# Step 0 of a fused attention and two-layer kernel: order of weight loads, weight splitting, gram evictions and the second half's solve

## The reference, cut to what matters

```python
k_n = k / (norm(k) + 1e-6)                       # batch 4, heads 8, 768 tokens, head size 48
for t in range(768):
    y[t] = q[t] @ state
    state += beta[t] * outer(k_n[t], v[t] - k_n[t] @ state)
x = y as (3072 tokens, 384)
h = x @ w_in                                     # 384 -> 2048
g = where(h >= 1, h, where(h <= -1, 0, (h + 1)**2 / 4))
x = g @ w_out                                    # 2048 -> 384
xn = x / rms(x) * rms_g                          # second network: 384 -> 1536 -> 384, silu gate
out = (silu(xn @ w_gate) * (xn @ w_val)) @ w_out2
```

## Time and profile before

| what | value |
|---|---|
| median of 3 runs | 1063.65 us (1062.71 to 1069.65) |
| the profiled execution's own time | 1068.47 us |
| its span from first to last instruction | 1066.6 us |
| mean granted TensorE clock | 0.99 |
| TensorE busy | 1039.2 us, 97% |

### The profile page before, as it was taken

How to read it: one execution, slowest core, us unless ns; L and a number is a source line. 1 busy time by engine, 2 the same in 40 slices (tenths; PEclk the granted TensorE clock), 3 DMA queues, 4 the chain that set the end, 5 groups by cost and what they waited for, 6 DMA issues and landing times.

```text
span 1066.6 us, 25024 instructions
## 1 busy us (share of the span) xinstructions
PE 1039.2 (97%) x11132; PEld 856.3 (80%) x11132; DVE 535.0 (50%) x1001; ACT 468.8 (44%) x843; POOL 9.6 (1%) x20
## 2 busy tenths in 40 slices
PE   8889899999999999999999999999999999999996
PEld 4469888777777877777778888888888888888885
DVE  6648667747846837753356444324333333333322
ACT  5744654574473474464466542232232232232211
POOL 1000000000000000000000000000000000000000
PEclk9889999999999999999999999999999999999999
DMA  9405102301500410030021230200200100100101
GB/s 258 133 2 130 22 3 62 89 3 37 115 2 3 120 31 3 32 119 3 28 93 49 70 119 1 60 1 1 60 1 13 48 1 1 30 1 1 30 1 30
DMA packets 19034, 48.09 MB, mean 45 GB/s; under 512 B 2448, under 2 KB 9232, under 8 KB 17872
## 3 DMA queue, kind: packets, MB, share of 16 engines
q1 hardware_dynamic: 18800, 46.11, 16.0%
q10 hardware_dynamic: 128, 0.39, 0.1%
HBM read 37.06 MB, written 9.44 MB: 44 GB/s over the span
## 4 chain that ended last, share of the span: by engine, by line
PE 92%; ACT 3%; DMA 2%; issue 1%; DVE 1%; SPq 0%; DVEq 0%; ACTq 0%
PE bank L713 21%; PE hps L1257 19%; PE acc L1272 19%; PE acc L732 10%; PE hps L713 7%; PE hps L732 4%; DMA stage<-w_in 1%; PE acc L1294 1%; PE bank L1216 1%; PE bank L1151 1%; PE bank L1180 1%; PE bank L1202 1%; PE bank L1195 1%; PE bank L1229 1%; PE bank L1141 1%
## 5 line engine op out<-in xcount | busy, mean ns | idle before, releaser
L630 ACT ACTIVATE g<-bank 128x512 f32<-128x512 f32 x72 | 43.2, 600 | 257.2 <-PE bank L713 142.6
L1257 PE MATMUL hps<-xh,w1h 128*128 128x512 f32 (+1 forms) x336 | 129.5, 385 | 2.7 <-DVE g L1089 2.1
L1272 PE MATMUL acc<-g1h,w2h 128*128 128x512 f32 (+1 forms) x336 | 127.0, 378 | 0.4 <-ACT x2s L941 0.3
L1257 PE MATMUL hps<-xl,w1h 128*128 128x512 f32 (+1 forms) x336 | 122.4, 364 | 0.0
L1257 PE MATMUL hps<-xh,w1l 128*128 128x512 f32 (+1 forms) x336 | 122.2, 364 | 0.0
L1272 PE MATMUL acc<-g1l,w2h 128*128 128x512 f32 (+1 forms) x336 | 122.0, 363 | 0.0
L1272 PE MATMUL acc<-g1h,w2l 128*128 128x512 f32 (+1 forms) x336 | 121.8, 363 | 0.0
L933 ACT ACTIVATE g1h<-g 128x512 fp32r<-128x512 f32 (+1 forms) x112 | 64.0, 571 | 120.6 <-DVE g L1089 105.5
L1097 DVE TENSOR_TENSOR g1l<-g,g1h 128x512 fp32r<-128x512 f32 (+1 forms) x112 | 68.6, 612 | 91.5 <-ACT g1h L933 91.1
L1089 DVE SCALAR_TENSOR_TENSOR g<-hps,g 128x512 f32<-128x512 f32 (+1 forms) x112 | 68.2, 609 | 61.6 <-ACT g L927 61.4
L924 ACT ACTIVATE g<-hps,half_c 128x512 f32<-128x512 f32 (+1 forms) x112 | 69.8, 623 | 54.0 <-PE hps L1257 53.2
(11 more groups left out here) (183 smaller groups left out, 2039.9 us busy)
## 6 DMA issues: line engine op xcount, KB each, us to landing
kqT<-kq SPq DMA_DIRECT2D x22, 384.0 KB, 6.6
v_in<-v SPq DMA_DIRECT2D x6, 768.0 KB, 4.3
k_in<-k SPq DMA_DIRECT2D x6, 768.0 KB, 5.6
x2d<-x2s SPq DMA_DIRECT2D x18, 256.0 KB, 5.2
x2t<-x2d SPq DMA_DIRECT2D x6, 768.0 KB, 5.5
y<-y_t SPq DMA_DIRECT2D x48, 96.0 KB, 2.2
stage<-w_in SPq DMA_DIRECT2D x4, 768.0 KB, 9.9
stage<-w_out SPq DMA_DIRECT2D x4, 768.0 KB, 7.6
```

The source lines that it names most:

```text
L630: act.activation(silu[:, f % 2, :], gps[f % 2][:, :], ACT.Silu).then_inc(e_silu, 1)
L1257: last = pe.matmul(hps[f % 2][:, 0:WIDTH[n]], wt[:, kk, P * f:P * f + P], xx[:, kk, COLS[n]], start=(kk == 0 and e == 0), stop=(kk == KD - ...
L1272: last = pe.matmul(acc[j][:, 0:WIDTH[n]], wt[:, f, P * j:P * j + P], gg[:, f % 2, 0:WIDTH[n]], start=(f == 0 and e == 0), stop=(f == NF1 - ...
```

## The change

It touches step 0 alone.

- Six chunks instead of four can be in flight: chunk 4 is loaded into `k_in` and chunk 5 into the query half of step 1's buffer. Chunks 0 to 5 are issued in a row, then the keys of step 1, then chunks 6 and 7 (which wait for the low parts of chunks 0 and 1), then queries and values. `k_in` is loaded once the low parts of chunk 4 are done, step 1's queries once those of chunk 5 are.
- 4 warm-up products instead of 6, and `hi` of chunk 0 before `nrm` instead of after.
- 21 pieces before `ft` instead of 18; pieces 21, 22 and 23 lie between the entries of the solve, and none in the network.
- The grams of step 1 are evicted one bank per entry (GE), with low parts between.
- Z(0,1) moves behind U(0,0), X(0,1) into the network after unit 3, directly ahead of its eviction. X(0,0)'s eviction is shared: ScalarE two operations, VectorE two (XB), and U(0,0) waits for both. `up`(0,1) and the second scaling of the values (`vnh`) come before the network.
- KU(0,0) after unit 6 in banks 2 and 0, KS(0,1) after unit 9. `trh`(1,0), which was in the first list, comes after unit 7.

```diff
-BESIDE = 18
+BESIDE = 21
-    out = [("warm", 0, 2), ("GK", 0, 0), ("GK", 0, 1), ("warm", 0, 6)]
+    out = [("warm", 0, 2), ("GK", 0, 0), ("GK", 0, 1), ("warm", 0, 4)]
+            ev += {13: [("GK", 1, 0)], 14: [("GE", 1, 0)], 15: [("GE", 1, 1)], 16: [("GK", 1, 1)], 17: [("GE", 1, 2)], 18: [("GE", 1, 3)],
+                   20: [("GQ", 0, 0)]}.get(p, [])
+        if e[0] == "nrm":
+            out += [("hi", 0, 0), e, ("hi", 0, 1)]
+            continue
-    out += low(16) + low(17)
-    out += [("ft", 0, 0), ("up", 0, 0), ("Z", 0, 0), ("Z", 0, 1), ("xd", 0, 0)] + piece(18) + [("X", 0, 0), ("X", 0, 1)]
-    out += [("vnh", 0, 0), ("GQE", 0, 0), ("hi", 0, 7), ("U", 0, 0)] + piece(19) + [("trh", 1, 0)] + low(18)
-    out += [("PU", 0, 0)] + piece(20) + low(19) + [("XT", 0, n) for n in range(KD)] + piece(21)
-    out += [("XE", 0, n) for n in range(KD)] + low(20) + low(21)
-    return out, inversion(1)[1:]
+    out += low(19) + low(20) + [("ft", 0, 0), ("up", 0, 0), ("Z", 0, 0), ("ZE", 0, 0), ("xd", 0, 0)] + piece(21) + low(21)
+    out += [("X", 0, 0), ("vnh", 0, 0), ("XB", 0, 0), ("GQE", 0, 0)] + piece(22) + low(22) + [("U", 0, 0), ("Z", 0, 1), ("ZE", 0, 1)]
+    out += [("vnh", 0, 1), ("PU", 0, 0)] + piece(23) + [("XT", 0, n) for n in range(KD)] + low(23)
+    out += [("XE", 0, n) for n in range(KD)] + [("up", 0, 1)]
+    return out, inversion(1)
-    return [(1, ("piece", 0, 22)), (2, ("piece", 0, 23)), (2, ("vnh", 0, 1)), (3, ("low", 0, 22)), (3, ("low", 0, 23)),
-            (3, ("up", 0, 1)), (3, ("XD", 0, 1)), (5, ("KU", 0, 0)), (8, ("KS", 0, 1)), (11, ("GQ", 0, 1)), (11, ("GQE", 0, 1)),
+    return [(3, ("X", 0, 1)), (3, ("XD", 0, 1)), (6, ("KU", 0, 0)), (9, ("KS", 0, 1)), (12, ("GQ", 0, 1)), (12, ("GQE", 0, 1)),
-                        if n >= NSTAGE:
-                            sp.wait_ge(s_wl, PIECES * (n - NSTAGE + 1))
-                        sp.dma_start(stage_as(n), w_chunk(w1_src, w2_src, n)).then_inc(s_w[n % NSTAGE], 16)
+                        if n >= NSTAGE + 2:
+                            sp.wait_ge(s_wl, PIECES * (n - NSTAGE - 1))
+                        sp.dma_start(stage_as(n), w_chunk(w1_src, w2_src, n)).then_inc(s_w[n], 16)
-                    for n in range(NSTAGE - 1):
+                    for n in range(NSTAGE + 2):
                         load_w(n)
                     load_kq(1, (0,))
-                    load_w(NSTAGE - 1)
-                    load_w(NSTAGE)
+                    for n in range(NSTAGE + 2, NCHUNK):
+                        load_w(n)
+                    load_kq(0, (1,))
                     load_v(0)
-                    load_kq(0, (1,))
-                    for n in range(NSTAGE + 1, NCHUNK):
-                        load_w(n)
+                    sp.wait_ge(s_wl, PIECES * (NSTAGE + 1))
                     load_k(0)
+                        elif kind == "XB":
+                            dve.wait_ge(p_x, half(c, q))
+                            dve.wait_ge(s_up, half(c, q))
+                            for e in range(MEM):
+                                last = dve.tensor_scalar_mul(tt[block_rows(1, 0), every_other(q, e), BLK:C],
+                                                             crossing(("X", c, q), block_rows(1, e)), -1.0)
+                            last.then_inc(s_xb, 1)
```

More of the change, by code:

```diff
@@ L95 @@
 NPIECE = NCHUNK * PIECES
-BESIDE = 18
+BESIDE = 21
 def first_body():
-    out = [("warm", 0, 2), ("GK", 0, 0), ("GK", 0, 1), ("warm", 0, 6)]
-    pieces = list(range(NPIECE))
+    out = [("warm", 0, 2), ("GK", 0, 0), ("GK", 0, 1), ("warm", 0, 4)]
+    done = 0
     def split(n):
         ev = []
-        for p in pieces[:n]:
+        for p in range(done, done + n):
             ev.append(("piece", 0, p))
@@ L111, in split @@
                 ev.append(("low", 0, p - 2))
-            if p % PIECES == 1 and 2 <= p // PIECES + 1 < NCHUNK - 1:
+            if p % PIECES == 1 and 2 <= p // PIECES + 1 < NCHUNK:
                 ev.append(("hi", 0, p // PIECES + 1))
-        del pieces[:n]
+            ev += {13: [("GK", 1, 0)], 14: [("GE", 1, 0)], 15: [("GE", 1, 1)], 16: [("GK", 1, 1)], 17: [("GE", 1, 2)], 18: [("GE", 1, 3)],
+                   20: [("GQ", 0, 0)]}.get(p, [])
         return ev
@@ L119, in first_body @@
             break
+        if e[0] == "nrm":
+            out += [("hi", 0, 0), e, ("hi", 0, 1)]
+            continue
         out.append(e)
-        if e[0] == "nrm":
-            out += [("hi", 0, 0), ("hi", 0, 1)]
         if e[0] == "inv":
-            out += split(BESIDE * (e[2] + 1) // INV - BESIDE * e[2] // INV)
-            out += {13: [("GK", 1, 0)], 18: [("GK", 1, 1)], 24: [("GQ", 0, 0)]}.get(e[2], [])
+            n = BESIDE * (e[2] + 1) // INV - done
+            out += split(n)
+            done += n
     def piece(p):
@@ L222 @@
 NPSUM = NBANK + 2 + KD
-FIRST = {("GK", 0, 0): (0, 1), ("GK", 0, 1): (3, 4), ("GK", 1, 0): (0, 3), ("GK", 1, 1): (4, 0), ("GQ", 0, 0): (1, 2),
-         ("Z", 0, 0): (0,), ("Z", 0, 1): (3,), ("X", 0, 0): (4,), ("X", 0, 1): (0,), ("U", 0, 0): (3, 4),
-         ("PU", 0, 0): (1, 2), ("XT", 0, 0): (3,), ("XT", 0, 1): (4,), ("XT", 0, 2): (2,), ("KU", 0, 0): (1, 0)}
+FIRST = {("GK", 0, 0): (0, 1), ("GK", 0, 1): (3, 4), ("GK", 1, 0): (0, 3), ("GK", 1, 1): (4, 2), ("GQ", 0, 0): (1, 0),
+         ("Z", 0, 0): (3,), ("X", 0, 0): (4,), ("U", 0, 0): (2, 3), ("Z", 0, 1): (4,), ("PU", 0, 0): (1, 0),
+         ("XT", 0, 0): (3,), ("XT", 0, 1): (2,), ("XT", 0, 2): (0,), ("X", 0, 1): (1,), ("KU", 0, 0): (2, 0)}
 def banks():
@@ L439, in build @@
             s_k0 = sem("first_keys_loaded")
+            s_xb = sem("cross_second_ready")
             s_gk2, s_upd2, s_y2 = sem("gram_second_ready"), sem("upd_second_ready"), sem("attn_y_second_ready")
             s_k, s_v, s_beta, s_kq = sem("k_loaded"), sem("v_loaded"), sem("beta_loaded"), [sem_pair("k_turned_loaded"), sem_pair("q_turned_loaded")]
-            s_w = [sem(f"w_loaded{i}") for i in range(NSTAGE)]
+            s_w = [sem(f"w_loaded{i}") for i in range(NCHUNK)]
             s_const0, s_const, s_neg = sem("const_zeroed"), sem("const_ready"), sem("negative_ready")
@@ L532, in w_piece, with stage_of @@
                 return t2[:, :, :].rearrange("p f n -> p (f n)")[:, f0:f0 + 512]
+            def stage_of(n):
+                if n == NSTAGE:
+                    return k_in[:, :, :].rearrange("p i d -> p (i d)")
+                if n == NSTAGE + 1:
+                    return kqT[1][:, 1, :, :].rearrange("p i t -> p (i t)")[:, 0:SPLIT]
+                return stage[:, n % (NSTAGE + 2), :]
             def stage_as(n):
-                s = stage[:, n % NSTAGE, :]
+                s = stage_of(n)
                 if n < NCHUNK // 2:
@@ L800, in _ @@
                         if c == 1:
+                            sp.wait_ge(s_wl, PIECES * (NSTAGE + 2))
                             load_kq(1, (1,))
@@ L853, in attention @@
                         kind, c, hf = u
-                        if kind == "GK":
+                        if kind == "GE":
+                            u = ("GK", c, hf // NQH)
+                            j = hf % NQH
+                            act.wait_ge(p_gk, half(c, hf // NQH))
+                            act.activation(gram[c][:, H * hf:H * hf + H, :],
+                                           bank_of(u, j)[:, :].rearrange("p (i t) -> p i t", t=C), ACT.Copy).then_inc(s_gf, 1)
+                            act.wait_ge(s_gf, HALVES + hf + 1)
+                            for r in UPPER:
+                                last = act.activation(gram[c][r, H * hf:H * hf + H, BLK:C],
+                                                      bank_of(u, j)[r, :].rearrange("p (i t) -> p i t", t=C)[:, :, 0:BLK], ACT.Copy)
+                            last.then_inc(s_gk, 1)
+                        elif kind == "GK" and c != 1:
                             act.wait_ge(p_gk, half(c, hf))
@@ L880, in attention @@
                             act.activation(nrm[:, :], sys_diag, ACT.Sqrt).then_inc(s_nrm, 1)
-                        elif kind == "Z":
+                        elif kind == ("Z" if c else "ZE"):
+                            u = ("Z", c, hf)
                             act.wait_ge(p_z, half(c, hf))
@@ L890, in attention @@
                             act.wait_ge(s_up, half(c, hf))
-                            for m in range(MEM):
+                            for m in range(MEM if c or hf else 1):
                                 for e in range(MEM):
@@ L946, in split @@
                             n = p
-                            act.wait_ge(s_w[n % NSTAGE], 16 * (n // NSTAGE + 1))
+                            act.wait_ge(s_w[n], 16)
                             act.activation(w_chunk(w1h, w2h, n), stage_as(n), ACT.Copy).then_inc(s_wh, 1)
@@ L978, in attention @@
                                     dve.wait_ge(s_gk2, HALVES)
-                                else:
+                                if c:
```

(7 more changed lines are left out.)

## The result

The changed kernel takes 1059.18 us (median of 12 runs, 1058.11 to 1063.06) against 1063.7 us before (12 runs, 1062.71 to 1069.95): ratio 0.9946, 95% interval 0.9929 to 0.9963. By the medians it is faster by 4.5 us, 0.4%. The ratio, which takes in all runs, stands for some 5.7 us, since four of the 12 runs before lay at 1069.3 to 1070.0. Forecast were 1052.1 us, a gain of 11.5; the measured time lies inside the stated range of 1047 to 1060.

A forecast was written before the change was run, and what follows sets the result against it. TensorE, busy 97% of the span, was taken as the bound, with time to win only before 75 us. Terms: 4.9 + 3.4 + 5.9 - 1.5 - 1.2 = 11.5 us; 1063.65 - 11.5 = 1052.1 us, range 1047 to 1060.

The forecast's parts named there:

- start of `up`(0,0): First step of the solve on ScalarE: starts at 41.2 instead of 46.13 through earlier splitting of the weights, gain 4.9 us.
- from there to the first unit: From `up`(0,0) to the first network product: 10.0 us instead of 13.4, gain 3.4, network begins at 51.2.
- from there to unit 9, past KS(0,1): From the first network product to the end of KS(0,1): 8.0 us instead of 13.9, gain 5.9.
- given back: Losses set against the gains: 1.5 us for VectorE lagging after the solve, 1.2 for stretches at the lower clock.
- carried to the median: Last step of the sum: profiled execution is 4.8 us above the median; full 11.5 taken from 1063.65, giving 1052.1.
- The 6.1 us by which ScalarE's queue was late: Before the solve: `up`(0,0) starts at 46.13 though `ft` ends at 39.99; splitting weights in ScalarE's queue sets the start.
- the stop of 4.08 us: TensorE ahead of KU(0,0), at 63.66: waits for bank 0, held by X(0,1); the change was to remove it.
- VectorE takes it back: Rival, from 59 us on: VectorE and TensorE, both nearly full, wait for each other; price 6 instead of 1.5, 1056.6; chance 0.25.

The follow-up runs named there:

- both: Changed kernel with piece 23 ahead of PU(0,0) and X(0,1)'s eviction shared between ScalarE and VectorE: 1059.48 us, ratio 0.9943 to the kernel before.

## Why the prediction was wrong

By its own terms, in us. "Clean" is the second profile before (span 1061.9), which stands for most executions:

| term | forecast | first profile before to after | clean profile before to after |
|---|---|---|---|
| start of `up`(0,0) | 4.9 | 46.13 to 41.58: 4.6 | 43.35 to 41.58: 1.8 |
| from there to the first unit | 3.4 | 13.4 to 13.0: 0.4 | 11.8 to 13.0: -1.2 |
| from there to unit 9, past KS(0,1) | 5.9 | 14.2 to 8.3: 5.9 | 13.4 to 8.3: 5.1 |
| given back | -2.7 | -1.7 | -1.1 |
| sum | 11.5 | 9.2 | 4.5 |

Of the 7.0 us between 11.5 and 4.5, 4.7 lie between the two executions of the kernel before, and 2.3 between the forecast and the first profile before: 3.0 too few in the second term, 0.3 in the first, and 1.0 less given back than was set aside.

**The step that failed first** is the last line of the sum: "carried to the median, 1063.65 - 11.5 = 1052.1". The 4.8 us between that execution and the median were noticed and treated as lying outside the argument. They lay in it: stretches at 1.2 GHz between 28.9 and 56.2, of which two held up ScalarE (2.94 us for the products of a gram and 1.78 for a piece, against 1.38 and 1.43 in the clean profile), and one slowed PU. The 6.1 us by which ScalarE's queue was late were 2.8 in the clean profile (`ft` ends at 40.51, `up` starts at 43.35). In the seven executions of ten that are of the first kind there were some 1.8 us to win at that place, not 4.9.

**The step that failed second** is the second term, from `up`(0,0) to the network in 10.0 us. It took 13.0. Three terms were missing from it: 0.7 us of small gaps up to PU, 1.8 for PU's stop, and about 0.5 for the rest, in it the clock stretch from 52.5 on (piece 23 took 1.4 instead of 1.1). The stop was not in the list of rivals. Against the clean profile (11.8) the part that was to gain 3.4 us lost 1.2.

**What held.** The start of `up`(0,0) after the change (41.2 and 41.58). The third term, 8.0 forecast against 8.3 and 7.7 in the two profiles, with KU's stop gone and 1.2 us ahead of KS(0,1) instead of 1.6. Its reason was half right: the prediction read the stop of 4.08 us as a wait for bank 0 and named ScalarE's queue as what is late next; the run with other banks shows that the queue was the limit all along, and the run with `up`(0,1) put back that it still is. From chunk 2 on no engine waited for a transfer in step 0; ahead of that ScalarE waited 1.43 us for chunk 1, and `hi` of chunk 2 came at 16.60 where 15.7 was forecast. VectorE did not take the gain back: TensorE waited 2.4 us for `g` between 64 and 240, against 2.1 in the clean profile before. What is lost after unit 9 is idle time of TensorE: the waits listed from there to 240 add up to 6.7 us against 5.3, among them 3.0 against 2.2 for evictions of grams. Why they grew stays open; the plans of steps 2 to 5 are the same in both kernels. Of the rivals, "VectorE takes it back" (1056.6) was nearest in time, and its mechanism is not what happened.

**What the change lives from** is in the main one part of it: the 2.3 us of low parts and `up`(0,1) taken from ahead of `g1h`(0,0), with the two pieces placed to suit. Alone in the kernel before it gives 2.2 us; taking a little more than half of it out of the changed kernel costs some 3.7. The parts alone add up to 2.9 (2.2 and 0.7), so how the whole 4.5 divides is not shown: no run took the loads or the 21 pieces out of the changed kernel. That the loads in a row and the earlier splitting steady the clock (no run of 20 at 0.990 or less, against 17 of 83 before) is argued from the counts; the run with these alone speaks against it, with seven of its 12 runs at 0.990 or less.

## What to carry to other kernels

Before a gain is summed from one profiled execution, compare its time with the median: a difference of the size of the expected gain must be found in the rows first, and the granted clock of each window is where to look. A stop at a buffer is worth only what the next waiter in line does not take over; follow each queue that the released instruction feeds, and change one entry to test it. Idle time can cost more than itself through the clock: here a wait longer by 1.4 us was followed by 3.4 us at 1.2 GHz, and the profiled execution was 2.8 us longer.

## What was not expected of the hardware

- The time of one and the same program follows its mean granted clock: 59 runs at 0.993 or more with a median of 1063.8 us, 17 at 0.990 or less with 1069.1. In the two that were profiled the difference arose in the first 75 us (0.89 and 0.98 there).
- TensorE stopped for 1.5 to 2.1 us inside PU(0,0), in five profiles of five in which U, Z(0,1) and PU followed each other (192 products of 0.02 us pitch, each with its weight load), and for 0.4 to 0.7 us in the three in which three long products stood between Z(0,1) and PU. In the changed kernel one packet of 16 KB of the instruction queue moved between 48 and 52 us:

```profile
q8 instruction: 1, 0.02, 1.7%
...
48.50:49.00 0.50, 0.50 (x37) 1.00 0.14 33
```

It started at 48.9 and took 1.1 us (1.7% of 16 engines' 4 us), and TensorE went on at 51.40. The other profiles, with the times read the same way:

| profile | packet starts | takes | TensorE goes on | after the packet's end | stop |
|---|---|---|---|---|---|
| changed kernel | 48.88 | 1.10 | 51.40 | 1.4 | 1.81 |
| changed kernel again | 49.32 | 0.97 | 51.58 | 1.3 | 1.54 |
| `up`(0,1) put back | 49.25 | 0.96 | 51.51 | 1.3 | 2.09 |
| X(0,1) shared | 48.78 | 0.96 | 51.06 | 1.3 | 1.54 |
| grams in one go | 49.44 | 1.36 | 52.23 | 1.4 | 2.09 |
| piece 23 ahead of PU | 48.51 | 0.96 | 50.86 | 1.4 | 0.39 |
| the same again | 48.84 | 0.99 | 51.20 | 1.4 | 0.39 |
| both | 48.99 | 1.26 | 51.63 | 1.4 | 0.67 |

Long stop or short, TensorE goes on 1.3 to 1.4 us after the packet is through. That the stream of instructions ran dry and the stop ends with its refill fits all eight; no run changed the refill alone.
